# Reordering the first batch of a three-stage kernel: DMA issues, gate preparation and held-back matmuls

## The reference

```python
mag = sqrt(a_re**2 + a_im**2); scale = minimum(mag, 0.999) / (mag + 1e-6)
for t in range(S):                                  # B=4, H=8, S=768, D=48
    S_re, S_im = ar*S_re - ai*S_im + k[t]*v[t]^T, ar*S_im + ai*S_re
    y[t] = q[t] @ S_re
x = y as (B, S, 384)
h = relu(x @ w_in)                                  # 384 -> 1024
x = (h * sigmoid(conv3(h))) @ w_out                 # 1024 -> 384
per expert e of 4: softmax(causal(q k^T / 8)) v wo, summed over the two best experts of each token
```

## Time and profile before

| | |
|---|---|
| median of 3 runs | 761.46 us (760.39 to 762.34) |
| profiled execution, its own time | 762.34 us |
| its span in the profile | 760.4 us |
| TensorE busy | 668.8 us, 88% |
| VectorE (DVE) busy | 614.8 us, 81% |
| ScalarE (ACT) busy | 409.3 us, 54% |
| mean DMA share over the span, queue of SP | 31.7% |

### The profile page before, as it was taken

How to read it: one execution, slowest core, us unless ns; L and a number is a source line. 1 busy time by engine, 2 the same in 40 slices (tenths; PEclk the granted TensorE clock), 3 DMA queues, 4 the chain that set the end, 5 groups by cost and what they waited for, 6 DMA issues and landing times.

```text
span 760.4 us, 13280 instructions
## 1 busy us (share of the span) xinstructions
PE 668.8 (88%) x5274; PEld 509.3 (67%) x5274; DVE 614.8 (81%) x1165; ACT 409.3 (54%) x747; POOL 0.2 (0%) x4
## 2 busy tenths in 40 slices
PE   0007788799999999999999999999999999999998
PEld 0003677676656788876667788776666888998765
DVE  3999977999888878899888788999888675773563
ACT  6404337533767755434757656434756334654565
POOL 0000000000000000000000000000000000000000
PEclk9999989999999999999999999999999999999999
DMA  8604774300028563400029554200037440000001
GB/s 343 260 0 130 209 222 149 125 0 0 1 82 232 160 176 90 161 2 0 1 86 263 153 150 151 97 1 0 1 103 209 128 124 5 1 1 1 1 22 42
DMA packets 93629, 73.85 MB, mean 97 GB/s; under 512 B 8704, under 2 KB 85760, under 8 KB 92928
## 3 DMA queue, kind: packets, MB, share of 16 engines
q1 hardware_dynamic: 93568, 73.01, 31.7%
HBM read 49.34 MB, written 23.65 MB: 96 GB/s over the span
## 4 chain that ended last, share of the span: by engine, by line
PE 42%; DVE 38%; ACT 8%; DMA 6%; issue 3%; SPq 2%; DVEq 0%; ACTq 0%
DVE cv L1130 8%; PE wide L1561 5%; PE wide L1580 4%; PE wide L1425 4%; DVE m L948 3%; PE bank L1639 3%; PE bank L1631 3%; DVE heads L1135 3%; PE wide L1437 3%; PE wide L1615 3%; DVE nmax L1194 2%; DMA araw<-a_in 2%; DMA heads_dram<-araw 2%; DVE m L947 2%; PE wide L1556 2%
## 5 line engine op out<-in xcount | busy, mean ns | idle before, releaser
L1490 PE MATMUL wide<-x_hi_lo,win_hi 128*128 128x384 f32 x384 | 109.1, 353 | 9.0 <-ACT h L657 4.9
L1490 PEld LDWEIGHTS wide<-x_hi_lo,win_hi 128*128 128x128 f32 x384 | 70.8, 190 | 13.6 <-issue 6.0
L1194 DVE TENSOR_REDUCE nmax<-wide 128x1 f32<-128x768 f32 (+2 forms) x96 | 55.2, 617 | 23.4 <-PE wide L1589 23.2
L1511 PE MATMUL wide<-heads,wout 128*128 128x384 f32 x200 | 70.6, 496 | 3.4 <-DVE heads L1135 3.4
L1130 DVE SCALAR_TENSOR_TENSOR cv<-h,wconv,cv 128x768 f32<-128x768 f32 x64 | 64.8, 1013 | 8.2 <-ACT cv L679 6.6
L1580 PE MATMUL wide<-attn 64*128 64x512 f32 (+3 forms) x256 | 65.0, 482 | 2.3 <-ACT attn L703 2.3
L727 ACT ACTIVATE xs<-wide 128x896 f32<-128x896 f32 x48 | 44.0, 917 | 41.7 <-PE wide L1615 41.7
L1490 PE MATMUL wide<-x_hi_lo,win_lo 128*128 128x384 f32 x192 | 65.1, 339 | 0.0
L684 ACT ACTIVATE cv<-cv 128x768 f32<-128x768 f32 x32 | 27.1, 846 | 57.7 <-DVE cv L1130 57.4
L1399 PE MATMUL wide<-attn,ident 128*128 128x512 f32 x4 | 3.1, 860 | 62.2 <-ACT m L621 62.2
L1511 PEld LDWEIGHTS wide<-heads,wout 128*128 128x128 f32 x200 | 36.3, 189 | 29.8 <-DVE heads L1135 9.9
(11 more groups left out here) (205 smaller groups left out, 1512.3 us busy)
## 6 DMA issues: line engine op xcount, KB each, us to landing
heads<-heads_dram SPq DMA_DIRECT2D x96, 192.0 KB, 3.6
araw<-a_in SPq DMA_DIRECT2D x12, 768.0 KB, 6.3
araw<-qk_in SPq DMA_DIRECT2D x12, 768.0 KB, 4.8
heads_dram<-m SPq DMA_DIRECT2D x18, 384.0 KB, 3.5
heads_dram<-araw SPq DMA_DIRECT2D x18, 384.0 KB, 4.0
v<-v_in SPq DMA_DIRECT2D x4, 1536.0 KB, 6.6
out_dram<-h SPq DMA_DIRECT2D x24, 192.0 KB, 2.6
heads_dram<-m SPq DMA_DIRECT2D x12, 192.0 KB, 2.8
```

Of the source, the lines that this page charges most:

```text
L1194: dve.tensor_reduce(nmax[:, t, side:side + 1], slot_scores(t, side), AXX, ALU.max, negate=True).then_inc(s_nm, 1)
L1490: last = MM(low[u % 2][:, 0:NT], w[:, k, mt * P:(mt + 1) * P], xs[:, k, n * NT:(n + 1) * NT], start=(k == 0 and part == 0), stop=(k == KT ...
L1511: last = MM(mlp_bank[u][:, 0:NT], wout[:, mt, k * P:(k + 1) * P], hgate(mt)[:, n * NT:(n + 1) * NT], start=(mt == 0), stop=(mt == MT - 1))
```

## The change

Only the preparation ahead of batch 0 and batch 0 itself are touched.

- SP: `load_heads(0, 0)` goes ahead of `store_unit(0, 0)`, `store_first_chunk(1)` ahead of `store_decay(0)`, `load_heads(0, 2)` ahead of `load_decay(0)`. `load_a(1, 0)` goes from its place before `load_heads(0, 3)` to one behind it, and `load_a(1, 1)` from behind `store_first_chunk(2)` to ahead of it.
- ACT: the squares of units 0 and 1 of batch 1 go from chunks 2 and 3 to chunk 2, their magnitudes from chunk 4 to chunk 3, and the square, magnitude of unit 2 from the feed-forward layer into chunks 4 and 5, with their table loads.
- DVE: `decay(0)` goes behind `mask(0, 0)`; `inverse(0, 2)` ahead of `state_step(0, 0)`; both chunk products of unit 2 into chunk 0; the steps of batch 1 are spread over chunks 2 to 5, and `norm(1, 1)` goes ahead of the first `conv`.
- PE: `keep_busy(HOLD)` goes from behind `w_in_rest` to the beginning of chunk 1 of batch 0.

```diff
             store_first_chunk(0)
+            load_heads(0, 0)
             store_unit(0, 0)
-            load_heads(0, 0)
             load_heads(0, 1)
+            store_first_chunk(1)
             store_decay(0)
+            load_heads(0, 2)
             load_decay(0)
-            store_first_chunk(1)
-            load_heads(0, 2)
             store_unit(0, 1)
-            load_a(1, 0)
...
                 else:
+                    load_a(1, 0)
+                    load_a(1, 1)
                     store_first_chunk(2)
-                    load_a(1, 1)
                 load_heads(b, 4)
...
                     if b == 0:
-                        if c in (2, 3):
-                            squares(1, c - 2)
-                        if c == 4:
+                        if c == 2:
+                            squares(1, 0)
+                            squares(1, 1)
+                        if c == 3:
                             nc.scalar.preload_act_table_set("sqrt_and_others")
                             magnitude(1, 0)
                             magnitude(1, 1)
+                        if c == 4:
+                            squares(1, 2)
                             exp_tables()
                             ln(1, 0)
                             guess(1, 0)
                         if c == 5:
                             ln(1, 1)
                             guess(1, 1)
+                            nc.scalar.preload_act_table_set("sqrt_and_others")
+                            magnitude(1, 2)
+                            exp_tables()
                     copy_x(b, c)
...
-                    if b == mt == 0:
-                        squares(1, 2)
                     relu(b, mt)
...
                     if b == mt == 0:
-                        nc.scalar.preload_act_table_set("sqrt_and_others")
-                        magnitude(1, 2)
-                        exp_tables()
                         ln(1, 2)
                         guess(1, 2)
...
                         mask(b, c + 1)
+                        if b == c == 0:
+                            inverse(0, UNITS - 1)
                         state_step(b, c)
                     if c + 1 < GAINS:
                         state_sum(b, c + 1)
                     if b == 0:
                         if c == 0:
-                            inverse(0, UNITS - 1)
                             scale_qk(0, UNITS - 1)
-                        if c < UNIT_CHUNKS:
-                            products_by_chunk(UNITS - 1, c)
+                            for half in range(UNIT_CHUNKS):
+                                products_by_chunk(UNITS - 1, half)
                         if c == 2:
-                            clear_edges()
-                        if c == 3:
                             gate_sumsq(1, 0)
                             gate_sumsq(1, 1)
+                        if c == 3:
+                            clear_edges()
+                        if c == 4:
+                            gate_sumsq(1, 2)
+                            norm_step(1, 0, 0)
                         if c == 5:
-                            norm_step(1, 0, 0)
+                            norm_step(1, 0, 1)
+                            norm_step(1, 0, 2)
...
                 x_low(b, NC - 1)
-                if b == 0:
-                    gate_sumsq(1, 2)
-                    norm_step(1, 0, 1)
-                    norm_step(1, 0, 2)
+                if more and b == 0:
                     write_w(1, 0)
+                    norm(1, 1)
...
                     if b == 0 and mt == 0:
-                        norm(1, 1)
                         write_w(1, 1)
...
-                if u == 1:
-                    decay(0)
                 inverse(0, u)
...
                     mask(0, 0)
+                    decay(0)
                     state_sum(0, 0)
...
                 for c in range(NC):
+                    if b == 0 and c == 1:
+                        keep_busy(HOLD)
...
-            keep_busy(HOLD)
```

## The result

The changed kernel takes 768.56 us (median of 20 runs, 765.72 to 770.88) against 761.4 us of the kernel before (757.79 to 769.42, 20 runs). The ratio is 1.0095, 95% interval 1.008 to 1.0111: slower by 7.2 us. The forecast was 3.5 us slower, range 760.5 to 767.6. The direction was right, the size was half of what came. The profiled execution has 768.12 us and a span of 766.2.

What follows compares the result with a forecast made beforehand. Bound by the DMA queue, then ACT's copies, up to VectorE reaching gate_h(0, 0). Queue +1.9, last gate load now waited for +1.1, tail +0.5: +3.5 us, 765.0 us on the median 761.46, range 760.5 to 767.6.

Steps and rivals of the forecast that it cites:

- Where the time is decided: VectorE reaching gate_h(0, 0), 139.97 us before: a shift of this moment passes to the end one for one.
- The term of the queue: SP's DMA queue: store_first_chunk(2) lands at 104.4 instead of 102.54, +1.9 us, behind both gate loads.
- the first of SP's moves: load_heads(0, 0) ahead of store_unit(0, 0): first scores come 1 to 2 us sooner, worth nothing as VectorE is busy.
- The decay's wait: VectorE's state_step(0, 0): the moved inverse(0, 2) hides nearly the whole wait for load_decay, at most 1 us left.
- From the landing to the last gate load: SP's queue behind the stores keeps order and intervals, so load_a(1, 2) lands at 121.9 instead of 120.04.
- ACT's list: ACT from squares(1, 2), waiting for its load until 121.9: x_low(5) ends 12.1 us later, at 134.0 instead of 127.85.
- VectorE and the tail: Behind x_low(5), 8.9 us of VectorE work remain to gate_h(0, 0), plus 0.5 us waiting for ACT's sigmoid.
- the drain of the Trainium skill: Rival on ACT: table switches cost 2.66 us, 1.38 of it drain; three add 4.1 us, giving 769.1; chance 0.02.
- The ring's order: DMA engines consume one issuer's descriptors in order, so both gate loads go wholly before the stores; otherwise +1.9 us becomes 0.
- A: Rival in SP's queue: the gate loads don't hold up the stores, first term 0, 763.1 us; chance 0.20.
- B: Rival: stores land 1.4 us sooner with both loads ahead, squares(1, 2) start at 116.4, 758.9 us; chance 0.15.
- C: Rival: delays add up, load_decay late by 3.5 us, stores land at 106.2, 766.8 us, up to 768; chance 0.10.

Runs made afterwards that it cites:

- e4: Kernel before with only both gate loads moved directly ahead of store_first_chunk(2) on SP: 768.24 us, ratio 1.0097.
- e1: Changed kernel with both gate loads back in their old places on SP: 764.79 us, ratio 1.0043.
- e5: Changed kernel with load_a(1, 0) alone back ahead of load_heads(0, 3): 769.01 us, ratio 1.0100.
- e6: Changed kernel with load_a(1, 1) alone back behind store_first_chunk(2): 765.96 us, ratio 1.0078.
- e12: Changed kernel with SP order, decay(0), idle products and unit 2's gate preparation as before, except load_heads(0, 0) still ahead of store_unit(0, 0): 764.21 us, ratio 1.0039.
- e2: Changed kernel with SP's order up to store_unit(0, 1) and the place of decay(0) as before: 768.21 us, ratio 1.0093.
- e11: Kernel before with only SP's new order from store_first_chunk(0) to store_unit(0, 1) and decay(0) behind mask(0, 0): 763.17 us, ratio 1.0008.
- e9: Changed kernel with gate loads back in old places and unit 2's gate preparation back in the feed-forward layer: 762.57 us, ratio 1.0009.
- e3: Changed kernel with the gate preparation of unit 2 of batch 1 back in the feed-forward layer: 765.48 us, ratio 1.0061.
- e8: Changed kernel with SP order, decay(0), idle products and unit 2's gate preparation of batch 1 all as before: 759.66 us, ratio 1.0002.
- e10: Changed kernel with unit 2's gate preparation back in the feed-forward layer and six more idle products ahead of scores(4): 765.86 us, ratio 1.0056.

## Why the prediction was wrong

**Where the time is decided: right.** `gate_h(0, 0)` stands 6.8 us later and VectorE behind it is as full as it was. That a shift passes to the end one for one is nearly right: 5.8 of 6.8 do.

**The term of the queue: mis-sized, and this is the step that failed.** The landing of the stores of unit 2 was forecast to be 1.9 us later; it is 6.4 us later.
- The prediction counted "the remainder of that load, the heads of chunk 3, the stores and the second load" as four transfers that had all landed by 104.3, and so a new order of the same four as nearly free. They are not the same four. Before, the first load was moved while SP waited for stores to land and while the heads, already issued, had not begun to move: 0.64 of its 0.79 MB were through when the first packet of the heads moved. Behind the heads, the load leaves this hole empty (share 0.19) and is moved whole, with the second, directly ahead of the stores. An estimate from the packets: 1.57 - 0.15 = 1.42 MB more gates ahead of the stores, at the 275 GB/s of 96 to 104 us, are 5.2 us, and the heads' first packet is 1.1 us later (95.40 against 94.28); together 6.3. e4 shows the price of this move alone, e1 its return, e5 and e6 about 2 us of passage for each load.
- The stores were forecast to be issued "when they were", and are issued 2.5 us later. The prediction left out that the two loads must be issued ahead of them, 1.3 us (e4 has the same 1.3, 96.54 against 95.21, with its heads of chunk 3 at their old 93.31). The other 1.1 us come with `load_heads(0, 3)`: it goes out at 94.44, forecast was 92.5. Ahead of it `load_decay` was issued at 89.0, not at 86.0 to 87.3, since the heads of chunk 2 waited for stores to land until 85.98 and took 2.99 us to be issued. In e12 the first of SP's moves, priced at 0 because it brings the first scores forward, delays these heads by 5 us, but in another order of SP's list; and in e2, which takes the whole early part back, the stores of unit 2 are issued no sooner than 97.46. So what makes these heads late in the changed kernel is not shown. The later issue is not an extra loss beside the bytes: in e11 it was 3.6 us later and the landing 2.3.

**The decay's wait.** At most 1 us was forecast, 2.39 measured; it lies on the way to the first issue. By e2 and e9 it is worth nothing that can be told in time.

**From the landing to the last gate load.** 17.5 us were forecast, 16.25 measured (108.92 to 125.17), so the load was 3.3 us later than forecast, not 4.5. Its landing took 6.38 us for 6.0.

**ACT's list: right.** `squares(1, 2)` waited for its load, though only by 0.38 us: `copy_x(3)` ended at 124.8, where 119.7 was forecast. And `x_low(5)` ended 12.2 us behind it (12.1 forecast). This list costs 0.0034, some 2.6 us of the result (e3, and e9 against e1). The table loads took 1.28 us each, and the next instruction followed within 0.02 us; the drain of the Trainium skill ("ScalarE: Activation LUTs", What ACT_TABLE_LOAD costs) was not seen here either.

**VectorE and the tail: right.** 9.4 us lie between `x_low(5)` and `gate_h(0, 0)`, 8.9 + 0.5 were forecast, with the 0.56 us of waiting for the sigmoid.

**The ring's order.** The Trainium skill ("DMA: Bandwidth & Descriptors", Queues, rings and completion order) says that on an engine descriptors of one issuer are consumed in ring order. The trace agrees: no packet of the stores moved from 99.1 to 103 us, while the two loads issued ahead of them did, and yet the second load landed at 106.8, after three of the four stores.

**The rivals.** A is excluded by e4. B needed the squares to start before 118.95; they started at 125.17. C had a part of the mechanism, a late decay and the transfers behind it further back, which is worth about 1.1 of the 6.4 us; its landing was 106.2. The sum with measured terms: 6.4 (landing) - 1.25 (queue behind it) + 1.1 + 0.1 (ACT's list) + 0.5 is 6.9, against 6.8 in the profile.

## What to carry to other kernels

An issue queue that waits for its own stores has holes, which in this kernel were some 2 to 4 us each. A long transfer that nobody waits for belongs into such a hole, behind stores that are about to be waited for, and not directly ahead of stores whose landing starts the next round trip. Its issuing counts too, 0.6 us a load here. To price a transfer in a queue, separate the time in which its bytes move from the time until its semaphore rises: the second can be filled by another transfer, the first can't. And before putting a step of preparation ahead of a copy that others wait for, look at when the step's own input lands.

## What the runs showed that was not expected

- The time that issuing takes varies: the last two stores of unit 2's first chunk took 2.74 us in the changed kernel, 1.44 before. A full queue can't be the only reason, since the heads of chunk 2 took 2.99 and 2.96 us at a DMA share of 0.3 to 0.5, where those of chunk 3 took 1.86.
- The length of a low-clock stretch varied. TensorE ran at 1.2 GHz behind gaps of 2 us and more ahead of scores(4). Around them the granted clock was 0.50 for 3 us in the kernel before (gap 1.97), 7 in the changed one (5.93), 10 in e4 (6.59) and 14 in e5 (3.61); behind gaps of 1.17 (e1), 1.41 (e8) and 1.51 (e12) it stayed at full clock in that chunk. In e9 and e10 it was low for nearly 14 us from 83 on.
- Single executions of one kernel differ by several us (757.79 to 769.42 for the kernel before), so a profile's span 5 us shorter (e8) was no gain in time.
